# Attention stage of a fused block on one Trainium2 core: an accumulator copy shared between two engines, and a value product moved ahead of the transposes

## The reference

```python
q_pool = q.reshape(B, H, S // factor, factor, D).mean(axis=3)
scores = scale * np.matmul(q_pool, k.transpose(0, 1, 3, 2))
scores = scores - np.max(scores, axis=-1, keepdims=True)
attn = np.exp(scores)
attn = attn / (np.sum(attn, axis=-1, keepdims=True) + 1e-09)
return np.matmul(attn, v).astype(np.float32)
```

## Time and profile before

| | |
|---|---|
| runs | 1007.09, 1007.63, 1009.69 us, median 1007.63 |
| the profiled execution | 1007.09 us, its span 1005.0 us |
| granted TensorE clock | 0.997 |
| PE busy | 985.4 us, 98% of the span |
| DVE busy | 568.5 us, 57% |
| ACT busy | 464.0 us, 46% |
| POOL busy | 382.8 us, 38% |
| chain that ended last | PE 92%, issue 2%, DVE 2%, POOL 1%, ACT 1%, DMA 1% |

### The profile page before, as it was taken

How to read it: one execution, slowest core, us unless ns; L and a number is a source line. 1 busy time by engine, 2 the same in 40 slices (tenths; PEclk the granted TensorE clock), 3 DMA queues, 4 the chain that set the end, 5 groups by cost and what they waited for, 6 DMA issues and landing times.

```text
span 1005.0 us, 22892 instructions
## 1 busy us (share of the span) xinstructions
PE 985.4 (98%) x8898; PEld 813.9 (81%) x8898; DVE 568.5 (57%) x1125; ACT 464.0 (46%) x880; POOL 382.8 (38%) x297
## 2 busy tenths in 40 slices
PE   6999999999999999999999999999999999999998
PEld 6877777777777777679999999988888888888898
DVE  6777777777777777779484948554213113121121
ACT  4787777777777877754242514222111111111111
POOL 4877777777777777730000104385000000000000
PEclk8999999999999999999999999999999999999999
DMA  5644444444444434310000000142001001000010
GB/s 184 182 119 118 117 117 117 116 112 114 116 117 117 117 91 109 111 55 1 1 2 1 2 1 24 46 135 73 1 0 42 1 1 42 0 15 27 0 42 22
DMA packets 34475, 65.55 MB, mean 65 GB/s; under 512 B 6272, under 2 KB 15360, under 8 KB 34432
## 3 DMA queue, kind: packets, MB, share of 16 engines
q1 hardware_dynamic: 33984, 64.37, 22.5%
q10 hardware_dynamic: 448, 0.56, 0.2%
HBM read 42.93 MB, written 4.72 MB: 47 GB/s over the span
## 4 chain that ended last, share of the span: by engine, by line
PE 92%; issue 2%; DVE 2%; POOL 1%; ACT 1%; DMA 1%; SPq 0%; DVEq 0%; ACTq 0%; POOLq 0%
PE ps L816 18%; PE ps L817 18%; PE ps L818 18%; PE ps L775 14%; PE ps L759 11%; PE ps L704 7%; PE ps L742 1%; DVE prob L1313 1%; PE ps L743 1%; PE ps L744 1%; PE ps L868 1%; DMA k_raw<-in_k 1%; ACT prob L1095 1%; POOL prob L592 0%; PE ps L822 0%
## 5 line engine op out<-in xcount | busy, mean ns | idle before, releaser
L1313 DVE TENSOR_SCALAR_CACHE_REDUCE prob<-ps 128x1152 f32<-128x1152 f32 x144 | 195.4, 1358 | 82.0 <-PE ps L759 62.8
L592 POOL TENSOR_SCALAR prob<-prob,rsum 128x1152 f32<-128x1152 f32 x144 | 178.4, 1239 | 106.0 <-DVE rsum L1322 106.0
L1095 ACT ACTIVATE prob<-prob,nmax 128x1152 f32<-128x1152 f32 x144 | 181.2, 1258 | 5.2
L775 PE MATMUL ps<-pT,v_sb 128*64 128x288 f32 x1152 | 170.6, 418 | 1.3
L1554 DVE SCALAR_TENSOR_TENSOR f_l<-ps,f_h 128x512 fp32r<-128x512 f32 (+1 forms) x60 | 38.3, 638 | 222.4 <-ACT f_h L1262 222.4
L1262 ACT ACTIVATE f_h<-ps 128x512 fp32r<-128x512 f32 (+1 forms) x60 | 33.3, 555 | 254.7 <-PE ps L818 254.7
L1081 ACT ACTIVATE pT<-ps 128x512 f32<-128x512 f32 (+1 forms) x288 | 111.9, 435 | 78.0 <-PE ps L704 69.4
L759 PE MATMUL ps<-k_over,q_over 64*128 64x288 f32 x744 | 131.5, 309 | 0.0
L759 PEld LDWEIGHTS ps<-k_over,q_over 64*128 64x128 f32 x744 | 102.1, 184 | 26.4 <-DVE prob L1313 25.8
L704 PE MATMUL ps<-ident,prob 64*128 64x64 f32 x2592 | 106.8, 224 | 6.7 <-DVE prob L1313 3.9
L704 PEld LDWEIGHTS ps<-ident,prob 64*128 64x128 f32 x2592 | 100.7, 139 | 13.8 <-issue 12.8
(11 more groups left out here) (156 smaller groups left out, 2136.9 us busy)
## 6 DMA issues: line engine op xcount, KB each, us to landing
q_raw<-in_q SPq DMA_DIRECT2D x16, 640.0 KB, 5.2
k_raw<-in_k SPq DMA_DIRECT2D x16, 576.0 KB, 4.0
v_sb<-in_v SPq DMA_DIRECT2D x32, 288.0 KB, 2.9
k_over<-kh SPq DMA_DIRECT2D x31, 144.0 KB, 2.5
k_over<-kl SPq DMA_DIRECT2D x31, 144.0 KB, 2.6
out_x<-xT SPq DMA_DIRECT2D x4, 1024.0 KB, 4.2
q_over<-qh SPq DMA_DIRECT2D x31, 128.0 KB, 2.2
q_over<-ql SPq DMA_DIRECT2D x31, 128.0 KB, 2.3
```

Of the source, the lines that this page charges most:

```text
L592: g.tensor_scalar(sl, sl, rsum[:, s:s + 1], 0.0, ALU.mult, ALU.add).then_inc(norm_done, 1)
L775: ins = te.matmul(ps[PH * c:PH * c + PH, ACC_BANK, 0:n], v_sb[:, a, j, :], pT[:, a, j, c * n:c * n + n], start=(j == 0), stop=(j == KB - 1))
L1095: sc.activation(sl, sl, ACT.Exp, scale=-1.0, bias=nmax[:, s:s + 1], accum_out=esum[:, s:s + 1]).then_inc(exp_done, 1)
L1313: ve.tensor_scalar(prob[:, PROB_BUF[s], :].rearrange("p (c n) -> p c n", c=SCORE_BANKS), ps[:, b0:b0 + SCORE_BANKS, 0:CK], -SCALE, BIG, AL ...
```

## The change

Four things change.

1. The semaphore `acc_moved` becomes two, `acc_by_act` and `acc_by_dve`. Of the two parts of bank 7, ScalarE copies the lower 64 partitions and VectorE the upper 64. VectorE's copy stands in steps 3 and 8 behind the reciprocal and ahead of take.
2. All that waited for `acc_moved` waits for both new semaphores.
3. In step 8, TensorE does values ahead of transpose_p. In all other steps the order stays.
4. `pT_free` is called once for a tile, at its head. For s = 4 ScalarE now waits ahead of its first copy and not between its two. For s = 5 the wait asks for the product of head 1, as for s = 4.

```diff
+        def pT_free(eng, i, s):
+            if s == 0 and not (isinstance(i, int) and i == 0):
+                eng.wait_ge(acc_ready, at(i, 4, -2))
+            if s in (TAIL_STEP, TAIL_STEP + 1) and not (isinstance(i, int) and i == 0):
+                eng.wait_ge(acc_ready, at(i, 4, 0))
...
@@ values, TensorE
-                        pe.wait_ge(acc_moved, at(i, 4, 2 * a))
+                        pe.wait_ge(acc_by_act, at(i, 2, a))
+                        pe.wait_ge(acc_by_dve, at(i, 2, a))
@@ step, TensorE
+                pv_first = s == NS - 1
+                if pv_first and not first:
+                    values(i - 1, *PV_STEPS[s])
                 if s >= LAG and not tail:
...
                     transpose_p(i, s - LAG)
...
-                if not first:
+                if not pv_first and not first:
                     values(i - 1, *PV_STEPS[s])
@@ evac_p and acc_copy, ScalarE
-                if s in (0, TAIL_STEP + 1):
-                    pT_free(act, i, head_of(s))
+                pT_free(act, i, s)
                 copy(pT_of(s, 0), trans(0)).then_inc(pT_by_act, 1)
-                if s == TAIL_STEP:
-                    pT_free(act, i, 1)
...
-                for c in range(2):
-                    copy(xT[PH * a:PH * a + PH, i, c * HALF:(c + 1) * HALF],
-                         ps[PH * c:PH * c + PH, ACC_BANK, 0:HALF]).then_inc(acc_moved, 1)
+                copy(xT[PH * a:PH * a + PH, i, 0:HALF], ps[0:PH, ACC_BANK, 0:HALF]).then_inc(acc_by_act, 1)
@@ VectorE
+            def acc_copy(i, a):
+                dve.wait_ge(acc_ready, at(i, 4, 2 * a + 2))
+                ve.tensor_copy(xT[PH * a:PH * a + PH, i, HALF:SQ], ps[PH:P, ACC_BANK, 0:HALF]).then_inc(acc_by_dve, 1)
@@ step, VectorE
+                if not first and s in (TAIL_STEP - 1, NS - 1):
+                    acc_copy(i - 1, 0 if s == TAIL_STEP - 1 else 1)
                 if not tail:
                     take(i, s)
@@ after attention, VectorE
-            dve.wait_ge(acc_moved, 4 * NP)
+            acc_copy(NP - 1, 1)
```

More of the change, by code:

```diff
@@ L244, in build @@
         acc_ready = sem("acc_ready")
-        acc_moved = sem("acc_moved")
+        acc_by_act = sem("acc_by_act")
+        acc_by_dve = sem("acc_by_dve")
         sgT_hi = sem("sgT_hi")
@@ L422, in first_bank @@
             return SCORE_BANKS * (s % 2) if s < LAG else 0
-        def pT_free(eng, i, a):
-            if not (isinstance(i, int) and i == 0):
-                eng.wait_ge(acc_ready, at(i, 4, 2 * a - 2))
+        def pT_free(eng, i, s):
[3 more added lines that the diff above has]
+                eng.wait_ge(acc_ready, at(i, 4, 0))
         def load_two(eng, rows):
@@ L519, in _ @@
                 load_w(u)
-            sp.wait_ge(acc_moved, 4 * NP)
+            sp.wait_ge(acc_by_act, 2 * NP)
+            sp.wait_ge(acc_by_dve, 2 * NP)
             sp.dma_start(b_row[:, :], b_sg.partition_broadcast(P)).then_inc(small_in, 16)
@@ L655, in _ @@
             norm_rstd(0, 1)
-            pool.wait_ge(acc_moved, 4 * NP)
+            pool.wait_ge(acc_by_act, 2 * NP)
+            pool.wait_ge(acc_by_dve, 2 * NP)
             for u in range(U_WO, U_T1):
@@ L833, in v_tile @@
                     if b == 0:
-                        pe.wait_ge(acc_moved, 4 * NP)
+                        pe.wait_ge(acc_by_act, 2 * NP)
+                        pe.wait_ge(acc_by_dve, 2 * NP)
                     pe.wait_ge(res_done, 4 * b + RES_N - 1)
@@ L1326, in evac_p @@
                 dve.wait_ge(p_ready, at(i, 2 * NS, 2 * s + 2))
-                if s in (0, TAIL_STEP, TAIL_STEP + 1):
-                    pT_free(dve, i, head_of(s))
+                pT_free(dve, i, s)
                 ve.tensor_copy(pT_of(s, 1), trans(1)).then_inc(pT_by_dve, 1)
+            def acc_copy(i, a):
+                dve.wait_ge(acc_ready, at(i, 4, 2 * a + 2))
+                ve.tensor_copy(xT[PH * a:PH * a + PH, i, HALF:SQ], ps[PH:P, ACC_BANK, 0:HALF]).then_inc(acc_by_dve, 1)
             def step(i, s, first=False, tail=False):
```

## The result

The change makes the kernel slower: 1014.42 us median of six runs (1012.8 to 1016.03) against 1008.76 of six (1007.09 to 1009.69), ratio 1.0054, 95% interval 1.0041 to 1.0067. I had forecast 1010.5, with 1014.0 as the upper end. Of the 3.9 us between forecast and result 1.1 come from the base, since the six runs of the kernel before have a median of 1008.76 where I had worked with 1007.63 of three; the growth is 5.7 us where I had 2.9. The profiled execution took 1012.23 us, 5.1 more than that of before, its span 1010.4 us.

A forecast was written before the change was run, and what follows sets the result against it. TensorE's own streaming was taken to bound the attention loop, except at steps 4 and 0. 15 pairs x (0.17 order + 0.03 copy) = 3.0 us on the profiled 1007.09 gave 1010.1, set at 1010.5 against run medians; range 1007.3 to 1014.0.

The forecast's parts named there:

- What bounds the kernel: Attention loop: TensorE streams its own work except at step 4, set by VectorE's take, and step 0, waiting 0.11 us.
- Step 8 in the new order: Scores of step 7 to transposes of step 0: 3.84 us instead of 3.67, evacuation having less cover; 0.17 a pair.
- Case B: Step 8: the new order is free on TensorE, +0.01 us a pair; 1008.2 us in all, chance 0.20.
- A rule and the rows: Step 8: if only a change of matmul kind costs, the new order costs TensorE nothing; same-kind rows say otherwise, 0.11 us.
- The shared copy, step 3: VectorE's 0.45 us copy ahead of take(3) delays the scores of step 4 by 0.03 us, bounds 0 and 0.15.
- The shared copy, step 8: VectorE's copy makes take of step 8 0.4 us late, covered by 12 value matmuls, so no cost.
- Step 0, bank 7: Value product of step 0 is not delayed by VectorE's copy, by 0.05 us only; bounds 0 and 0.15.
- All else of the change is waits already fulfilled: 0: Rest of the change, beyond the order and the copies: its waits are already fulfilled and cost 0.
- Rival D: VectorE's copy is the new wait, 0.15 us late in step 3 and step 0: 7 us, 1014.6; chance 0.22.
- The range: Whole kernel: 1007.3 to 1014.0 us.

The follow-up runs named there:

- e1: Kernel before with the bank 7 semaphore split in two, ScalarE still copying both parts; ratio 1.0007 to the kernel before, pair time 25.646 us.
- e5: Changed kernel with the step-3 copy back on ScalarE, VectorE copying its part in step 8 only; ratio 1.0040 to the kernel before, pair time 25.850 us.
- e17: Changed kernel with the parts of bank 7 exchanged, VectorE copying the lower 64 partitions; ratio 1.0039 to the kernel before, pair time 25.840 us.
- e16b: Changed kernel with one semaphore for bank 7, one for the evacuations, and the step-3 copy back on ScalarE; ratio 1.0023 to the kernel before, pair time 25.697 us.
- e15b: Changed kernel with one semaphore for bank 7 and one for the evacuations; ratio 1.0043 to the kernel before, pair time 25.805 us.
- e11: Changed kernel with both engines counting their bank 7 copies on one semaphore; ratio 1.0044 to the kernel before, pair time 25.844 us.
- e7b: Changed kernel with both bank 7 copies of step 8 moved ahead of the evacuation; ratio 1.0049 to the kernel before, pair time 25.960 us.
- e12: Kernel before without two repeated evacuation waits ahead of a head's first value product in the loop; ratio 0.9997 to the kernel before, pair time 25.520 us.
- e3: Kernel before with the new order on TensorE alone, ScalarE copying both parts; ratio 1.0050 to the kernel before, pair time 25.815 us.
- e18: Kernel before with VectorE copying the lower part of bank 7, one semaphore, old order, old place of waits; ratio 1.0001 to the kernel before, pair time 25.562 us.
- e13: Changed kernel without two evacuation waits ahead of a head's first value product; ratio 1.0047 to the kernel before, pair time 25.893 us.

## Why the prediction was wrong

The terms of a pair. The last three are each from two kernels that differ in that alone; the first is what is left of the changed kernel when they are taken away. So the sum is 0.426 by construction and no check of its own; the checks are e1 for the third term (0.110), e5 and e17 for the second (0.112, 0.122).

| term | from | measured, us | predicted |
|---|---|---|---|
| new order, evacuation with less cover | e16b less before | 0.161 | 0.17 |
| VectorE's copy ahead of take(3) | e15b less e16b | 0.108 | 0.03 |
| second semaphore for bank 7 | after less e11 | 0.118 | 0 |
| second semaphore of the evacuation, in even pairs | e11 less e15b | 0.039 | 0 |
| sum | | 0.426 | 0.20 |

15 x 0.426 is 6.4 us (5.4 in the spans), 15 x 0.20 was my 3.0.

- **What bounds the kernel**: right. TensorE streams in all steps but 4 and 0, and the loss is at these two, with 0.03 in step 8.
- **Step 8 in the new order**: right, in its parts as well. Scores to product 0.99 (0.99 forecast), to transposes 1.12 (1.13), last transpose to evacuation 216.14 - (215.30 + 0.78 - 0.22) = 0.28 (0.29), ScalarE's copies 0.77, to the transposes 0.14 (0.11). Sum 3.86 against 3.84. In even pairs 0.09 more came from the second semaphore. Case B, by which the order is free, is refuted: 0.161. But TensorE's own part of step 8 grew by only 0.03 (2.66 to 2.69); the rest is the evacuation that now ends later. And one reading against case B was wrong: I took 0.11 from the last transpose to scores of the same kind, from the first pair, and after the change it is 0.03 in all 15 step 8s, less than the 0.15 from a last transpose to a value product, where the kind changes. At this place a change of instruction within one kind so costs next to nothing, as the rule in "A rule and the rows" had it.
- **The shared copy, step 3**: the step that failed by size. Its length was right (0.46 for 0.45). The lengths of the gaps were not: I let the copy start 0.03 behind the reciprocal and take up to 0.08 before its end, as is the custom between others. It was 0.06 and 0.03 behind. The first is the register row and the wait row ahead of the copy, which the short reciprocal does not cover; e17 shows the cause for the second, the start partition of the copy's read. The term measured 0.108 for my 0.03; the bound of 0.15 held.
- **The shared copy, step 8**: right. Take(8) was 0.6 us late (I had 0.4) and cost nothing; e7b shows it.
- **Step 0, bank 7**: right that the copy does not gate (e7b), by a small margin: 0.03 in odd pairs, I had 0.05.
- **"All else of the change is waits already fulfilled: 0"**: the step that failed outright, and with 0.16 a pair the largest miss. The wait is fulfilled, but it needs a row of its own in TensorE's queue, and a row takes 0.106 us. Ahead of the value product of step 0 the queue has no lead, since 18 short transposes have just been issued (e1, e7b). The second 0.04 is the same row ahead of the transposes behind even pairs; that wait did exist before, and only the late end of ScalarE's evacuation brought it onto the path. I had read 0.71 against 0.64 in the earlier trace rows as the price of such rows, which it is not (e12), and used it only for the scores of step 8. The one place where I wrote of the added semaphore was step 4, where it shares a row and adds none.
- **Rival D** had nearly the right total, 1014.6, and half the right reason. Its other half, bank 7, is refuted by e11 and e7b. That the total fits is luck: the 0.157 of the semaphores stands where D had 0.15 for bank 7.
- **The range** left out an error of this kind: the bounds were for the copy alone. It was missed by 0.4 us, and with the base at 1007.63 the same growth would have ended inside it. That too would have been luck.

Not settled: the 0.03 by which e1 pays more than the changed kernel in step 0, and why the waits of one and the same line are packed into one row in one half of the loop body and into two in the other.

## What to carry to other kernels

Where the engine that bounds waits at the head of a stretch of long work behind many short instructions, count the rows of its queue, not only what they wait for. A wait that shares a row is free, one that needs a new row is not, and how the waits are packed shows in the queue rows of the trace. Where no engine can run ahead and fill the count for another, let all producers of one event count on one semaphore. Before covering work is moved, ask what it covers: the value product stood between the transposes and their next turn and hid two evacuations. And an engine's free 0.45 us does not take an operation of 0.45 us, if that has to start or end without the usual overlap.

## What the runs showed of the hardware

- A row with a fulfilled wait took 0.106 us of TensorE's queue, and no semaphore row carried more than two waits (the traces before and after). A second, fulfilled semaphore ahead of a matmul so cost 0.11 to 0.12 us a time where the queue had no lead and the wait needed a new row (e1, e11, e7b), and nothing where it shared a row (step 4 of e1). One row less in the kernel before gained 0.01 (e12). The Trainium skill, page "Perfetto Trace Analysis", section "Identifying Dependency Chains", says that instructions which wait for several engines may get separate semaphore instructions ahead of them; these runs agree and add the price.
- Two semaphores that both come late cost some 0.1 more than one where their waits stood in two rows (behind even pairs), and nothing more where they shared one (odd pairs; e11 against e15b).
- From a copy's end to the matmuls that it releases it was 0.10 to 0.15 us (before, e3, e16b, e18), and 0.24 where one more row of the queue stood between (e13).
- VectorE overlapped a copy and the operation behind it by at least 0.05 us when both read PSUM and wrote SBUF from partition 0, and left 0.03 between them when the copy read or wrote from partition 64 (e17, and the changed kernel).
